# One core, attention and two MLPs: the first MLP in token chunks of 512, 256, 512, 512, 512 instead of four of 464 and one of 448, with one tanh buffer

## The chip, the cores and the metric

The kernel runs on one core of a Trainium2 chip. The metric is the device time of one execution in microseconds; the median of three runs is 832.08 (832.0 to 832.1).

## What is computed

The reference, cut to what matters, with inputs q, k, v (4, 8, 576, 64), s (4, 8, 576) and all in float32:

```python
def _attn_ref(q, k, v, s):
    scores = np.matmul(q, k.transpose(0, 1, 3, 2)) / np.sqrt(D)
    cum = np.cumsum(np.maximum(s, 0.0), axis=-1)
    bias = -(cum[:, :, :, None] - cum[:, :, None, :])
    scores = np.where(causal, -1e9, scores + np.minimum(bias, 0.0))
    attn = softmax(scores)
    return np.matmul(attn, v)

def _moe_ref(x, w_in, w_out):           # 2304 tokens, 512 -> 2048 -> 512
    h = x @ w_in
    g = h - np.tanh(h)
    return g @ w_out

def _moe2_ref(x, w_in, w_out, g_ln):    # 2304 tokens, 512 -> 1024 -> 512
    h = x @ w_in
    solu = h * softmax(h)
    ln = (solu - mean(solu)) / np.sqrt(var(solu) + 1e-6) * g_ln
    return ln @ w_out
```

The output of the attention, 4 x 576 = 2304 tokens of 512 features, goes through the first MLP (`_moe_ref`, MLP1 below) and then the second.

## The kernel before

All data of the MLPs stays in SBUF with features on the partitions: `xT` holds the 2304 tokens as four blocks of 128 features. Every product in full precision is made of three float32r matmuls, high x high, low x high and high x low, where the high part is a copy rounded to float32r (ACT) and the low part is what is left (DVE, sometimes POOL).

**MLP1** goes over the tokens in five chunks (`NCH`): with `CH = 464` (line 76) four chunks of 464 tokens and a last one of 448. The hidden layer has `FT` = 16 blocks of 128 features; a step is one block j of one chunk c, and u = 16 c + j counts the steps. The program of each engine is written out by hand, and engines meet at semaphores only:

- TensorE: `up` (L1440 to L1452) makes one block of h, 12 matmuls into PSUM bank j % 4; `down` (L1454 to L1466) adds the block's share of the output to the four banks 4 to 7, 12 matmuls. Each matmul has its own weight load of 128x128. `chunk` (L1468) orders them: in chunk 0 `down(j - 4)` before `up(j)`, in the others `up(j)` before `down(j - 2)`. The first four `up` of chunk 0 are laid between the last matmuls of the attention (`first_up`, L1484).
- ACT, `step` (L836): tanh of the bank into `gate`, high part of the gate into `gate_hi`.
- DVE, `step` (L1130): h - tanh(h) into `gate` (L1134), low part into `gate_lo` (L1146).
- `gate`, `gate_hi` and `gate_lo` have two buffers each, taken in turn by j. Tanh of step u waits for `gate_lo` of step u - 2, since that reads the same `gate` last; `gate_hi` waits for the `down` of step u - 2:

```python
act.wait_ge(up_done, u + 1)
wait(act, gate_lo_done, u - 1)
act.activation(gate[j % 2][:, 0:wide(c)], h_ps[j % 4][:, 0:wide(c)], ACT.Tanh).then_inc(tanh_done, 1)
...
act.wait_ge(gate_done, u + 1)
wait(act, down_done, u - 1)
act.activation(gate_hi[j % 2][:, 0:wide(c)], gate[j % 2][:, 0:wide(c)], ACT.Copy).then_inc(gate_hi_done, 1)
```

Between chunks ACT and DVE split the next chunk's tokens (`split_x`, L799 and L1094: four high parts, four low parts), and copy the finished chunk's output from PSUM over the tokens in `xT` (`copy_y`, L970 and L1268). The first chunk's tokens are split by POOL (`first_x`, L667) while the attention still runs.

Other work is laid into the steps of two chunks. In chunk 0 ACT and DVE split the weights of MLP1, which SP loads through four staging tiles: in step j after the tanh the parts of `w1o` (L812, L1108), after `gate_hi` and `gate_lo` one part of `w1i` (L807, L1103). In the last chunk they split the weights of the second MLP: ACT the high part in step j between tanh and `gate_hi`, DVE the low part between the subtract and `gate_lo`. `W2_STEP` (L89) says which part is in which step: B22 in 5, B11 in 6, B21 in 7 (strided reads, two instructions of 512 per engine, L825 and L1120), then four sums T4, T2, T1, T3 in 9, 10, 11, 13 (L818, L1115) and the second layer's weights in 12, 14, 15. POOL makes the four sums (L702 to L714, eight instructions), starting when `down` of step 3 of the last chunk is done; when `down` of step 9 is done it splits the first two token tiles of the second MLP (`split_y`, L716).

The second MLP follows (L1657 to L1752): `up2` makes two token tiles by seven block products (42 matmuls of 512 columns), `turn_ln` transposes, `down2` makes the output. Its first `up2` stands ahead of the last two `down` of MLP1.

Loops: the middle chunks are a loop on the chip (`Fori`), the first and the last are straight code; on ACT and DVE the last but one as well.

In SBUF the gate tiles lie at the start of the phase's area, six of `CH` words (`GATE_W`), then `w1o`, `w1i`, and the split tokens `x_hi`, `x_lo` of 4 x `CH` words each. The second MLP's tiles lie over the same area.

Of the kernel before, what the change touches and what calls it, by code (L numbers as in the profile page):

```python
# [44 lines left out]
def wait(eng, sem, count):  # L45

    if not (isinstance(count, int) and count <= 0):
        eng.wait_ge(sem, count)


def build_transformer(nc, q, k, v, s, w_in, w_out, w2_in, w2_out, g_ln, out):
# [21 lines left out]
    FT = FF // P  # L73
    FF2 = w2_in.shape[1]
    FT2 = FF2 // P
    CH = 464
    NCH = -(-TOK // CH)
    LAST_CH = TOK - (NCH - 1) * CH
    TT = TOK // P
    assert D == 64 and TAIL == 64 and FULL == 4 and H % 2 == 0 and HALVES == KT == 4 and PAIRS % 2 == 0  # L80
    assert 0 < LAST_CH <= CH and LAST_CH % 16 == 0 and NCH > 3
    assert TT * P == TOK and TT % 4 == 2 and TT > 6 and FF2 == 2 * BANK and DM == BANK and FT2 == 8

    HK = KT // 2
# [39 lines left out]
    with ctx:  # L124
# [7 lines left out]
        g_col = sb("g_col", [P, FT2])  # L132


        GATE_W = 6 * CH
        attention_words = []
        with ExitStack() as phase:
            sb = tensors(phase, attention_words)
            qkT_hi = [sb(f"qkT_hi{n}", [P, QK_W], F32R) for n in range(2)]
            qkT_lo = [sb(f"qkT_lo{n}", [P, QK_W], F32R) for n in range(2)]  # L140
            probs = [sb(f"probs{n}", [P, PW]) for n in range(2)]
            pT_hi = sb("pT_hi", [P, 2, PT_W], F32R)

            v_parts = [sb(f"v_parts{n}", [P, NT, 4 * D], F32R) for n in range(2)]
            ident_b = sb("ident_b", [P, P], BF16)
            mask_b = sb("mask_b", [P, P], BF16)
            upper_b = sb("upper_b", [P, TAIL], BF16)
            lower_b = sb("lower_b", [P, TAIL], BF16)
            tail_mask_b = sb("tail_mask_b", [P, TAIL], BF16)
            neg_max = [sb(f"neg_max{n}", [P, TILES]) for n in range(2)]  # L150
            row_sum = [sb(f"row_sum{n}", [P, TILES]) for n in range(2)]
            den = [sb(f"den{n}", [P, TILES]) for n in range(2)]
            small_b = sb("small_b", [P, 1])
            rden = [sb(f"rden{n}", [P, TILES]) for n in range(2)]
            rden_row = sb("rden_row", [TILES, P])

            w1i_words = GATE_W + FT * 2 * DM
            sb("gap", [P, w1i_words - sum(attention_words)])
            cum_bc = [sb(f"cum_bc{n}", [P, 2, S]) for n in range(2)]
            cum_tail = sb("cum_tail", [P, S])  # L160
            v_raw = [sb(f"v_raw{n}", [P, NT, 2 * D]) for n in range(2)]
            pT_lo = sb("pT_lo", [P, 2, PT_W], F32R)
            rden_T = [sb(f"rden_T{n}", [P, S]) for n in range(2)]
            qk_flat = [sb(f"qk_flat{n}", [P, FULL * P]) for n in range(2)]
            x_low = sb("x_low", [P, S])
            x_sum = sb("x_sum", [P, S])
# [10 lines left out]

        AHEAD = 4
        behind_words = AHEAD * 2 * KT * P
        before = GATE_W + FT * 2 * DM  # L180
        pad = 0
        assert sum(attention_words) <= before + FT * 2 * KT * P - behind_words
        with ExitStack() as phase:
            sb = tensors(phase)
            gate = [sb(f"gate{n}", [P, CH]) for n in range(2)]
            gate_hi = [sb(f"gate_hi{n}", [P, CH], F32R) for n in range(2)]
            gate_lo = [sb(f"gate_lo{n}", [P, CH], F32R) for n in range(2)]
            w1o = sb("w1o", [P, FT, 2, DM], F32R)
            w1o_hi, w1o_lo = ([w1o[:, j, part, :] for j in range(FT)] for part in range(2))
            w1i = sb("w1i", [P, FT, 2, KT, P], F32R)  # L190
            w1i_hi, w1i_lo = ([w1i[:, (j - AHEAD) % FT, part, :, :] for j in range(FT)] for part in range(2))
            x_hi = sb("x_hi", [P, KT, CH], F32R)
            x_lo = sb("x_lo", [P, KT, CH], F32R)

        W1O_AT, W1I_AT = GATE_W, GATE_W + FT * 2 * DM
        mlp2_words = []
        with ExitStack() as phase:
            sb = tensors(phase, mlp2_words)  # L200
            out_sb = [sb(f"out_sb{n}", [P, DM]) for n in range(2)]
            sb("pad2", [P, W1O_AT - sum(mlp2_words)])
            w2o_a = sb("w2o_a", [P, 6, 2, DM], F32R)
            y_split_a = sb("y_split_a", [P, 2, 7, HK, P], F32R)
            y_sum = sb("y_sum", [P, 2, HK, P])
            act2 = [sb(f"act2_{n}", [P, FF2]) for n in range(2)]
            lnT_hi = [sb(f"lnT_hi{n}", [P, FT2, P], F32R) for n in range(2)]
            lnT_lo = [sb(f"lnT_lo{n}", [P, FT2, P], F32R) for n in range(2)]
            assert sum(mlp2_words) == W1I_AT
            w2x = sb("w2x", [P, FT, 2, BANK], F32R)  # L210
            y_split_b = sb("y_split_b", [P, 2, 7, HK, P], F32R)
            small = sb("small", [P, 64])
# [141 lines left out]

        def wide(c):

            return LAST_CH if isinstance(c, int) and c == NCH - 1 else CH

        def tokens(c):

            return slice(c * CH, c * CH + wide(c)) if isinstance(c, int) else bass.ts(c, CH)

        def w1o_at(j):

# [424 lines left out]
        def _(act):  # L789
# [46 lines left out]
            def step(c, j):  # L836
                u = FT * c + j
                act.wait_ge(up_done, u + 1)
                wait(act, gate_lo_done, u - 1)
                act.activation(gate[j % 2][:, 0:wide(c)], h_ps[j % 4][:, 0:wide(c)], ACT.Tanh).then_inc(tanh_done, 1)  # L840
                if isinstance(c, int) and c == 0:
                    for n in w1o_at(j):
                        w1o_hi_part(n)

                if isinstance(c, int) and c == NCH - 1:
                    for name in W2_STEP:
                        if W2_STEP[name] == j:
                            w2i_hi_part(name)
                    for f in W2O_STEP.get(j, ()):
                        w2o_hi_part(f)  # L850
                act.wait_ge(gate_done, u + 1)
                wait(act, down_done, u - 1)
                act.activation(gate_hi[j % 2][:, 0:wide(c)], gate[j % 2][:, 0:wide(c)], ACT.Copy).then_inc(gate_hi_done, 1)  # L853
                if isinstance(c, int) and c == 0 and 0 < j <= FT - AHEAD:
                    w1i_hi_part(j + AHEAD - 1)

# [113 lines left out]
            def copy_y(c):  # L970
                act.wait_ge(down_done, FT * (c + 1))
                for m in range(2):
                    act.activation(xT[:, m, tokens(c)], y_ps[m][:, 0:wide(c)], ACT.Copy).then_inc(y_act, 1)
# [8 lines left out]
                    act.wait_ge(x_done, PAIRS)  # L982
                step(0, j)
            split_x(1)
            with act.Fori(1, NCH - 2) as c:
                copy_y(c - 1)
                for j in range(FT):
                    step(c, j)
                split_x(c + 1)
            copy_y(NCH - 3)  # L990
            for j in range(FT):
                step(NCH - 2, j)
            split_x(NCH - 1)
# [81 lines left out]
        def _(dve):  # L1075
# [54 lines left out]
            def step(c, j):  # L1130
                u = FT * c + j
                dve.wait_ge(tanh_done, u + 1)
                n = wide(c)
                dve.tensor_tensor(gate[j % 2][:, 0:n], h_ps[j % 4][:, 0:n], gate[j % 2][:, 0:n],  # L1134
                                  ALU.subtract).then_inc(gate_done, 1)
                if isinstance(c, int) and c == 0:
                    for m in w1o_at(j):
# [1 line left out]
                if isinstance(c, int) and c == NCH - 1:  # L1139
# [3 lines left out]
                    for f in W2O_STEP.get(j, ()):  # L1143
                        w2o_lo_part(f)
                dve.wait_ge(gate_hi_done, u + 1)
                dve.tensor_tensor(gate_lo[j % 2][:, 0:n], gate[j % 2][:, 0:n], gate_hi[j % 2][:, 0:n].bitcast(F32),  # L1146
                                  ALU.subtract).then_inc(gate_lo_done, 1)
                if isinstance(c, int) and c == 0 and 0 < j <= FT - AHEAD:
                    w1i_lo_part(j + AHEAD - 1)
# [123 lines left out]
            for j in range(1, FT):  # L1273
                step(0, j)
            split_x(1)
            with dve.Fori(1, NCH - 2) as c:
                copy_y(c - 1)
                for j in range(FT):
                    step(c, j)
                split_x(c + 1)  # L1280
            copy_y(NCH - 3)
            for j in range(FT):
                step(NCH - 2, j)
            split_x(NCH - 1)
            copy_y(NCH - 2)
            for j in range(FT):
                step(NCH - 1, j)

# [143 lines left out]
        def _(pe):  # L1432
# [219 lines left out]

            pe.wait_ge(x_added, 2 * PAIRS)
            chunk(0, True)
            with pe.Fori(1, NCH - 1) as c:
                chunk(c, False)
            def up2(i, par, n, after):  # L1657

# [116 lines left out]
```

## Time and profile before

| | us |
|---|---|
| median of three runs | 832.08 |
| profiled execution | 825.32 |
| its span, first to last instruction | 823.5 |
| PE busy | 800.8 (97%) |
| DVE busy | 475.8 (58%) |
| ACT busy | 394.7 (48%) |
| POOL busy | 280.3 (34%) |
| attention, with the first weights (to 204.85) | 204.85 |
| MLP1, from its first matmul to the second MLP's second block (204.85 to 625.39) | 420.54 |
| rest of the second MLP (625.39 to 823.5) | 198.11 |

A row of a group names line, engine, operation, the tile written, the tiles read, the shapes and the count; "busy, mean ns" are the time of the group and of one instruction. A matmul's listed duration overlaps with the next one's, so the distance between starts is what one costs. The idle time of an engine stands with what released it.

### The profile page before, as it was taken

The page shows a single profiled execution, that of the slowest core. Times are in us where ns is not written, and L with a number is a line of the kernel's source. Part 1 is how long each engine was busy: PE and PEld are TensorE (multiplying, and loading weights), DVE is VectorE, ACT ScalarE, POOL GpSimd, SP SyncE. Part 2 cuts the span into 40 slices and gives each one's busy share as a digit, 9 for nine tenths or more (in the row PEclk, how much of TensorE's full clock was granted, in tenths as well). Part 3 has the DMA queues.
Part 4 walks back from the last instruction along what each step waited for, and adds up shares of the span by engine and source line. Part 5 has one row for each costly group of instructions (what it writes and reads, how often), then busy time and mean ns, then how long its engine had stood idle before and what let it go on. Part 6 is the DMA issues. An engine that isn't in the chain of part 4 may idle for free. (4 is left out here: it accounts for less than half of the span.)

```text
span 823.5 us, 14650 instructions
## 1 busy us (share of the span) xinstructions
PE 800.8 (97%) x4498; PEld 694.6 (84%) x4498; DVE 475.8 (58%) x1101; ACT 394.7 (48%) x935; POOL 280.3 (34%) x322
## 2 busy tenths in 40 slices
PE   6999999998999999999999999998999899999998
PEld 5888888887888888888888888897888788888886
DVE  5889888888854332233223322338678666666662
ACT  5999899888544332222222222325444443433433
POOL 3687787778100000000000000008274744444400
PEclk9999999999999999999999999999999999999999
DMA  7665555545433100000000000000200000000001
GB/s 184 149 154 159 143 137 154 144 114 145 138 113 110 65 1 0 1 1 0 0 0 0 0 0 0 0 1 1 102 1 1 27 25 27 14 25 25 13 25 51
DMA packets 77719, 46.34 MB, mean 56 GB/s; under 512 B 59824, under 2 KB 68144, under 8 KB 77680
## 3 DMA queue, kind: packets, MB, share of 16 engines
q1 hardware_dynamic: 75232, 45.19, 19.3%
q10 hardware_dynamic: 2448, 0.66, 0.4%
q8 instruction: 20, 0.33, 0.2%
q14 instruction: 19, 0.16, 0.1%
HBM read 40.97 MB, written 4.87 MB: 56 GB/s over the span
## 5 line engine op out<-in xcount | busy, mean ns | idle before, releaser
L1450 PE MATMUL psum<-x_hi,w1i 128*128 128x464 f32 (+1 forms) x640 | 185.7, 371 | 0.5 <-DVE w1i L1103 0.5
L1463 PE MATMUL psum<-gate_hi,w1o 128*128 128x464 f32 (+1 forms) x640 | 146.8, 371 | 3.3 <-DVE gate_lo L1146 3.3
L1463 PEld LDWEIGHTS psum<-gate_hi,w1o 128*128 128x128 f32 x640 | 119.9, 188 | 18.0 <-DVE gate_lo L1146 4.4
L1450 PEld LDWEIGHTS psum<-x_hi,w1i 128*128 128x128 f32 x640 | 119.7, 188 | 15.0 <-DVE w1i L1103 0.9
L1146 DVE TENSOR_TENSOR gate_lo<-gate,gate_hi 128x464 fp32r<-128x464 f32 (+1 forms) x80 | 56.4, 705 | 129.7 <-ACT gate_hi L853 129.7
L853 ACT ACTIVATE gate_hi<-gate 128x464 fp32r<-128x464 f32 (+1 forms) x80 | 47.1, 589 | 154.5 <-PE psum L1463 133.6
L706 POOL TENSOR_TENSOR w2t<-stage 128x512 f32<-128x512 f32 x2 | 4.8, 2442 | 338.0 <-PE psum L1463 338.0
L1450 PE MATMUL psum<-x_lo,w1i 128*128 128x464 f32 (+1 forms) x320 | 118.7, 371 | 0.0
L1134 DVE TENSOR_TENSOR gate<-psum,gate 128x464 f32<-128x464 f32 (+1 forms) x80 | 50.8, 636 | 94.2 <-ACT gate L840 94.1
L840 ACT ACTIVATE gate<-psum 128x464 f32<-128x464 f32 (+1 forms) x80 | 44.1, 551 | 101.7 <-PE psum L1450 97.2
L878 ACT ACTIVATE probs<-probs,neg_max 128x128 f32<-128x128 f32 (+2 forms) x144 | 83.7, 587 | 10.3 <-DVE neg_max L1179 10.0
L1162 DVE TENSOR_TENSOR pT_lo<-psum,pT_hi 128x512 fp32r<-128x512 f32 (+3 forms) x160 | 72.5, 477 | 14.2 <-ACT pT_hi L869 13.3
L1463 PE MATMUL psum<-gate_lo,w1o 128*128 128x464 f32 (+1 forms) x320 | 80.0, 371 | 0.0
L869 ACT ACTIVATE pT_hi<-psum 128x512 fp32r<-128x512 f32 (+3 forms) x160 | 64.2, 435 | 9.2 <-PE psum L1582 8.6
L1721 PE MATMUL psum<-w2o_a,lnT_hi 128*128 128x512 f32 x216 | 67.6, 394 | 0.2 <-DVE lnT_lo L1372 0.2
L1179 DVE CUSTOM_DVE_ANT_0 probs<-psum,cum_bc 128x128 f32<-128x128 f32 (+3 forms) x128 | 58.5, 481 | 13.9 <-PE psum L1510 10.5
L1450 PEld LDWEIGHTS psum<-x_lo,w1i 128*128 128x128 f32 x320 | 60.1, 188 | 6.7
L1463 PEld LDWEIGHTS psum<-gate_lo,w1o 128*128 128x128 f32 x320 | 60.1, 188 | 6.4
L1582 PE MATMUL psum<-ident,probs 128*128 128x128 f32 x400 | 60.4, 279 | 0.6 <-ACT probs L878 0.5
L1549 PE MATMUL psum<-pT_hi,v_parts 128*128 128x128 f32 (+2 forms) x192 | 56.2, 331 | 1.8 <-DVE x_sum L1202 1.3
L1688 PE MATMUL psum<-w2x,y_split_a 128*128 128x512 f32 x210 | 49.6, 392 | 0.0
L1582 PEld LDWEIGHTS psum<-ident,probs 128*128 128x128 f32 x400 | 45.3, 142 | 4.6 <-ACT qk_flat L904 1.7
(154 smaller groups left out, 1421.1 us busy)
## 6 DMA issues: line engine op xcount, KB each, us to landing
cum_bc<-cum_dram SPq DMA_DIRECT2D x16, 576.0 KB, 4.7
rden_T<-rden_dram SPq DMA_DIRECT2D x32, 144.0 KB, 3.0
out_x<-out_sb SPq DMA_DIRECT2D x18, 256.0 KB, 2.0
stage<-in_q SPq DMA_DIRECT2D x32, 128.0 KB, 2.4
v_raw<-in_v SPq DMA_DIRECT2D x32, 128.0 KB, 3.6
stage<-in_moe_w_in SPq DMA_DIRECT2D x16, 256.0 KB, 3.0
stage<-in_moe_w_out SPq DMA_DIRECT2D x16, 256.0 KB, 3.4
stage<-in_k SPq DMA_DIRECT2D x28, 128.0 KB, 2.3
```

Of the source, the lines that this page charges most:

```text
L869: hi = act.activation(to(pT_hi), ps, ACT.Copy)
L878: act.activation(probs[par][:, at:at + width], probs[par][:, at:at + width], ACT.Exp, bias=neg_max[par][:, col:col + 1], scale=-1.0, accum ...
L1134: dve.tensor_tensor(gate[j % 2][:, 0:n], h_ps[j % 4][:, 0:n], gate[j % 2][:, 0:n], ALU.subtract).then_inc(gate_done, 1)
L1146: dve.tensor_tensor(gate_lo[j % 2][:, 0:n], gate[j % 2][:, 0:n], gate_hi[j % 2][:, 0:n].bitcast(F32), ALU.subtract).then_inc(gate_lo_done, 1)
L1162: lo = dve.tensor_tensor(to(pT_lo), ps, to(pT_hi).bitcast(F32), ALU.subtract)
L1179: dve.tensor_tensor_reduce(probs[par][:, at:at + width], tail_bank(sl) if h is None else score_ps[h][t], cum_tail[:, :] if h is None else ...
L1450: mm = pe.matmul(h_ps[j % 4][:, 0:wide(c)], wp[j][:, kt, :], xp[:, kt, 0:wide(c)], start=(n == 0), stop=(n == 3 * KT - 1))
L1463: mm = pe.matmul(y_ps[m][:, 0:wide(c)], wp[j][:, m * P:(m + 1) * P], gp[j % 2][:, 0:wide(c)], start=(j == 0 and wp is w1o_hi and gp is gat ...
L1549: mm = pe.matmul(x_ps[:, c0:c1], v_parts[par][:, j, 2 * h * D:2 * h * D + P], pp[:, h, j * STEP + c0:j * STEP + c1], start=(j == 0 and n = ...
L1582: mm = pe.transpose(ps[:, n * P:(n + 1) * P], probs[par][:, at:at + P], ident[:, :])
L1688: mm = pe.matmul(h2_ps[n][at], yp[:, of, kt, :], wp[:, kt, :], start=(nth == at and kt == 0 and k == 0), stop=(last and kt == HK - 1 and k ...
L1721: mm = pe.matmul(out_ps[par], lp[par][:, f, :], wp[f][:, :], start=(f == 0 and n == 0), stop=(f == FT2 - 1 and n == 2))
```

## The change

The chunk width becomes 512, one PSUM bank, and the second chunk takes the 256 tokens that are left. `tokens` moves the start of every later chunk by 256. `gate` has one buffer, so that tanh of step u waits for `gate_lo` of step u - 1. The loops begin one chunk later: TensorE's chunk 1 is straight code and chunks 2 and 3 loop; on ACT and DVE chunks 0, 1 and 4 are straight code, and `copy_y(c)` moves from the start of the next turn of the loop to the end of its own. The gate area is five of 512 words, with 48 words of padding between `w1o` and `w1i`.

```diff
-    CH = 464
+    CH = BANK
     NCH = -(-TOK // CH)
-    LAST_CH = TOK - (NCH - 1) * CH
+    SHORT = TOK - (NCH - 1) * CH
...
-        GATE_W = 6 * CH
+        GATE_W, W1_PAD = 5 * CH, 48
...
-            gate = [sb(f"gate{n}", [P, CH]) for n in range(2)]
+            gate = sb("gate", [P, CH])
...
         def wide(c):
-            return LAST_CH if isinstance(c, int) and c == NCH - 1 else CH
+            return SHORT if isinstance(c, int) and c == 1 else CH
         def tokens(c):
-            return slice(c * CH, c * CH + wide(c)) if isinstance(c, int) else bass.ts(c, CH)
+            if not isinstance(c, int):
+                return bass.ds(c * CH - (CH - SHORT), CH)
+            at = c * CH - (CH - SHORT) * (c > 1)
+            return slice(at, at + wide(c))
...
             def step(c, j):
                 u = FT * c + j
                 act.wait_ge(up_done, u + 1)
-                wait(act, gate_lo_done, u - 1)
-                act.activation(gate[j % 2][:, 0:wide(c)], h_ps[j % 4][:, 0:wide(c)], ACT.Tanh).then_inc(tanh_done, 1)
+                wait(act, gate_lo_done, u)
+                act.activation(gate[:, 0:wide(c)], h_ps[j % 4][:, 0:wide(c)], ACT.Tanh).then_inc(tanh_done, 1)
...
             split_x(1)
-            with act.Fori(1, NCH - 2) as c:
-                copy_y(c - 1)
+            copy_y(0)
+            for j in range(FT):
+                step(1, j)
+            split_x(2)
+            copy_y(1)
+            with act.Fori(2, NCH - 1) as c:
                 for j in range(FT):
                     step(c, j)
                 split_x(c + 1)
-            copy_y(NCH - 3)
-            for j in range(FT):
-                step(NCH - 2, j)
-            split_x(NCH - 1)
-            copy_y(NCH - 2)
+                copy_y(c)
             for j in range(FT):
                 step(NCH - 1, j)
...
             chunk(0, True)
-            with pe.Fori(1, NCH - 1) as c:
+            chunk(1, False)
+            with pe.Fori(2, NCH - 1) as c:
                 chunk(c, False)
```

The same edits stand in DVE's program, and the padding once more in the second MLP's area.

## Rows read from the trace of the kernel before

**Rows 1.** Stages: start:end, us, busy us (count) by engine, PE clock, DMA, GB/s.

```profile
291.29:372.17 80.88, 80.88 (x386) 72.06 (x385) 23.97 (x38) 21.32 (x38) 0.00 (x0) 1.00 0.00 1
...
533.93:625.39 91.46, 88.13 (x427) 79.72 (x426) 61.12 (x72) 37.47 (x61) 41.39 (x33) 1.00 0.07 24
```

**Rows 2.** Waits of PE: us in total, times, longest us.

```profile
PE psum L1463 <- DVE gate_lo L1146: 3.3, 3, 1.7
...
PE psum L1450 <- DVE w1i L1103: 0.5, 1, 0.5
```

**Rows 3.** Timeline of PE, chunk 4: start, us; three steps apart.

```profile
589.10 1.76 PE L1463 MATMUL psum<-gate_hi,w1o 128*128 128x448 f32 x8
...
603.67 1.81 PE L1463 MATMUL psum<-gate_hi,w1o 128*128 128x448 f32 x8
```

**Rows 4.** Chain of waits in the second MLP: start, us, what.

```profile
722.68 6.82 PE psum L1688 x30
729.50 8.16 PE psum L1721 x36
737.66 0.87 PE psum L1704 x8
```

**Rows 5.** Timeline of PE in the attention, then the weight loads of L1524.

```profile
111.02 0.42 PE L1524 MATMUL psum<-qkT_hi 128*128 128x288 f32 x2
...
111.81 0.20 PE L1526 MATMUL psum<-tail_mask_b,ident_b 128*128 128x64 bf16 x1
...
113.07 0.25 PE L1549 MATMUL psum<-pT_hi,v_parts 128*128 128x192 f32 x1
...
113.28 0.21 PE L1549 MATMUL psum<-pT_hi,v_parts 128*128 128x64 f32 x1
...
L1524 PEld LDWEIGHTS psum<-qkT_hi,qkT_lo 128*128 128x128 f32 x32 | 5.2, 189 | 0.0
```

**Rows 6.** Groups by line and shape on ACT and DVE: busy us, mean ns, idle before.

```profile
L853 ACT ACTIVATE gate_hi<-gate 128x464 fp32r<-128x464 f32 x64 | 37.8, 591 | 130.8 <-PE psum L1463 122.9 <-DVE gate L1134 7.8
L840 ACT ACTIVATE gate<-psum 128x464 f32<-128x464 f32 x64 | 35.5, 554 | 81.7 <-PE psum L1450 79.0 <-DVE gate_lo L1146 2.7
...
L1146 DVE TENSOR_TENSOR gate_lo<-gate,gate_hi 128x464 fp32r<-128x464 f32 x64 | 41.1, 642 | 121.3 <-ACT gate_hi L853 121.3
L1134 DVE TENSOR_TENSOR gate<-psum,gate 128x464 f32<-128x464 f32 x64 | 40.9, 639 | 79.1 <-ACT gate L840 79.0
...
L1134 DVE TENSOR_TENSOR gate<-psum,gate 128x448 f32<-128x448 f32 x16 | 10.0, 622 | 15.1 <-ACT gate L840 15.1
```

**Rows 7.** Timeline of ACT, chunk 4, steps 5 and 6.

```profile
556.02 0.54 ACT L840 ACTIVATE gate<-psum 128x448 f32<-128x448 f32 x1 [1.78 <-PE psum L1450]
...
561.31 2.38 ACT L825 ACTIVATE w2x<-stage 128x512 fp32r<-128x512 f32 x2
```

**Rows 8.** Timeline of DVE, chunk 4, steps 5 to 7.

```profile
558.79 5.57 DVE L1120 TENSOR_TENSOR w2x<-stage,w2x 128x512 fp32r<-128x512 f32 x2 [1.57 <-ACT w2x L825]
564.28 2.02 DVE L1146 TENSOR_TENSOR gate_lo<-gate,gate_hi 128x448 fp32r<-128x448 f32 x1
...
566.77 4.54 DVE L1120 TENSOR_TENSOR w2x<-stage,w2x 128x512 fp32r<-128x512 f32 x2
571.24 1.90 DVE L1146 TENSOR_TENSOR gate_lo<-gate,gate_hi 128x448 fp32r<-128x448 f32 x1
...
578.60 0.62 DVE L1146 TENSOR_TENSOR gate_lo<-gate,gate_hi 128x448 fp32r<-128x448 f32 x1
```

**Rows 9.** Timeline of POOL, first and last of the sums.

```profile
558.57 4.84 POOL L706 TENSOR_TENSOR w2t<-stage 128x512 f32<-128x512 f32 x2 [337.96 <-PE psum L1463]
...
572.62 5.17 POOL L714 TENSOR_TENSOR w2t<-stage 128x512 f32<-128x512 f32 x2
```

**Rows 10.** Stages early in the attention, columns as in rows 1.

```profile
15.00:19.50 4.50, 2.34 (x27) 1.62 (x26) 2.61 (x8) 3.64 (x10) 2.28 (x3) 1.00 0.67 153
19.50:23.00 3.50, 3.50 (x20) 2.73 (x19) 2.87 (x15) 2.88 (x12) 2.24 (x4) 0.51 0.89 250
```

More of the change, by code:

```diff
@@ L75, in build_transformer @@
     FT2 = FF2 // P
-    CH = 464
+    CH = BANK
     NCH = -(-TOK // CH)
-    LAST_CH = TOK - (NCH - 1) * CH
+    SHORT = TOK - (NCH - 1) * CH
     TT = TOK // P
     assert D == 64 and TAIL == 64 and FULL == 4 and H % 2 == 0 and HALVES == KT == 4 and PAIRS % 2 == 0
-    assert 0 < LAST_CH <= CH and LAST_CH % 16 == 0 and NCH > 3
+    assert 0 < SHORT <= CH and SHORT % P == 0 and NCH == 5
     assert TT * P == TOK and TT % 4 == 2 and TT > 6 and FF2 == 2 * BANK and DM == BANK and FT2 == 8
@@ L155, in build_transformer @@
             rden_row = sb("rden_row", [TILES, P])
-            w1i_words = GATE_W + FT * 2 * DM
+            w1i_words = GATE_W + FT * 2 * DM + W1_PAD
             sb("gap", [P, w1i_words - sum(attention_words)])
@@ L179, in build_transformer @@
         behind_words = AHEAD * 2 * KT * P
-        before = GATE_W + FT * 2 * DM
+        before = GATE_W + FT * 2 * DM + W1_PAD
         pad = 0
@@ L189, in build_transformer @@
             w1o_hi, w1o_lo = ([w1o[:, j, part, :] for j in range(FT)] for part in range(2))
+            sb("pad1", [P, W1_PAD])
             w1i = sb("w1i", [P, FT, 2, KT, P], F32R)
@@ L193, in build_transformer @@
             x_lo = sb("x_lo", [P, KT, CH], F32R)
-        W1O_AT, W1I_AT = GATE_W, GATE_W + FT * 2 * DM
+        W1O_AT, W1I_AT = GATE_W, before
         mlp2_words = []
@@ L208, in build_transformer @@
             lnT_lo = [sb(f"lnT_lo{n}", [P, FT2, P], F32R) for n in range(2)]
+            sb("pad4", [P, W1_PAD])
             assert sum(mlp2_words) == W1I_AT
@@ L852, in step @@
                 wait(act, down_done, u - 1)
-                act.activation(gate_hi[j % 2][:, 0:wide(c)], gate[j % 2][:, 0:wide(c)], ACT.Copy).then_inc(gate_hi_done, 1)
+                act.activation(gate_hi[j % 2][:, 0:wide(c)], gate[:, 0:wide(c)], ACT.Copy).then_inc(gate_hi_done, 1)
                 if isinstance(c, int) and c == 0 and 0 < j <= FT - AHEAD:
@@ L1133, in step @@
                 n = wide(c)
-                dve.tensor_tensor(gate[j % 2][:, 0:n], h_ps[j % 4][:, 0:n], gate[j % 2][:, 0:n],
+                dve.tensor_tensor(gate[:, 0:n], h_ps[j % 4][:, 0:n], gate[:, 0:n],
                                   ALU.subtract).then_inc(gate_done, 1)
@@ L1145, in step @@
                 dve.wait_ge(gate_hi_done, u + 1)
-                dve.tensor_tensor(gate_lo[j % 2][:, 0:n], gate[j % 2][:, 0:n], gate_hi[j % 2][:, 0:n].bitcast(F32),
+                dve.tensor_tensor(gate_lo[j % 2][:, 0:n], gate[:, 0:n], gate_hi[j % 2][:, 0:n].bitcast(F32),
                                   ALU.subtract).then_inc(gate_lo_done, 1)
@@ L1275, in _ @@
             split_x(1)
-            with dve.Fori(1, NCH - 2) as c:
-                copy_y(c - 1)
+            copy_y(0)
+            for j in range(FT):
+                step(1, j)
+            split_x(2)
+            copy_y(1)
+            with dve.Fori(2, NCH - 1) as c:
                 for j in range(FT):
@@ L1280, in _ @@
                 split_x(c + 1)
[L1281 to L1285, printed above, removed]
+                copy_y(c)
             for j in range(FT):
```

## Prediction, made blind

> **What bounds the kernel now.** I read the stages first. The first MLP (MLP1) is one unbroken stretch of TensorE work: chunks 1, 2 and 3 take 80.88 us each (three rows alike, one shown) with PE busy for all of it, at a granted clock of 1.00, while DVE and ACT are busy for under a third [rows 1]. Each chunk holds 16 x 24 = 384 matmuls, so a 464-wide one costs 80.88/384 = 0.2106 us from start to start. Only chunk 4 shows PE short of its window (88.13 of 91.46) [rows 1]. The waits of PE name the cause: three waits for gate_lo in the down product, 3.3 us together; and one of 0.5 us for a w1i part in chunk 0 [rows 2]. So time moves by what one matmul costs at the new widths, and by what happens to the three stalls.
>
> **Matmul cost by width.** Four widths can be read as pitches.
> - 464: 0.2106 us (above).
> - 448: in the quiet part of chunk 4, three steps of 24 take 603.67 - 589.10 = 14.57 us, 0.2024 each [rows 3].
> - 512: in the second MLP 30 take 6.82 us (0.2273) and 36 take 8.16 us (0.2267) [rows 4]. I use 0.2270.
> - 256 appears with fp32 weights of 128x128 nowhere. Nearest above it: six of 288 take 111.81 - 111.02 = 0.79 us, 0.1317 each. Nearest below: two of 192 start in 113.28 - 113.07 = 0.21 us, 0.105 each [rows 5].
>
> The line through 288 and 512 rises (0.2270 - 0.1317)/224 = 0.000425 us per column; at 256 it gives 0.118. Bounds: not below the 192-wide 0.105, not above the 288-wide 0.1317. I take 0.119, near the line, because 288 is the closer of the two neighbours. The same line gives 0.2066 at 464 and 0.1998 at 448, so the present widths lie 0.0040 and 0.0026 above it: that excess is the whole of what can be won.
>
> **The change, part by part.**
>
> Chunks 0, 2, 3, from 464 to 512: each 384 x 0.2270 = 87.17, in place of 80.88, +6.29; three make +18.9. (Chunk 0 is mixed with the last attention work, but has the same 384 matmuls.)
>
> Chunk 1, from 464 to 256: 384 x 0.119 = 45.7 in place of 80.88, -35.2. By the bounds 40.3 to 50.6, so -5.4 to +4.9 around it.
>
> Chunk 4, from 448 to 512: 87.17 in place of 384 x 0.2024 = 77.7, +9.5.
>
> Together **-6.8 us**. A 512 pitch as high as 0.231 (the 464's extra 0.0040 added) would add 384 x 4 x 0.004 = 6.1.
>
> One tanh buffer. tanh of unit j now waits for gate_lo of j-1, not j-2; behind it on ACT stand gate_hi and, in chunks 0 and 4, the weight parts; DVE's subtract waits for it. Where nothing else is in the chain, tanh, subtract, gate_hi, gate_lo take 0.554 + 0.639 + 0.591 + 0.642 = 2.43 us at 464 [rows 6]; the step rate of PE is 24 x 0.2106 = 5.05. From 464 to 448 the subtract loses (639 - 622)/16 = 1.06 ns per column [rows 6]; with that for all four the chain is at most 2.63 at 512 against a step of 5.45, and about 1.55 at 256 against 2.86. Two further steps of slack stand behind it, since down(j) is issued after up(j+2). Cost zero in chunks 1 to 3; the cover is PE's step, and without it each step would cost the difference to the chain. In chunk 0 ACT has a w1o and a w1i part per step, but those still fit, and PE's longer first products cover part of the 0.5 us wait [rows 2]: I take -0.3, bounds -0.5 and +0.5.
>
> Boundary from chunk 1 to 2. Before it PE runs three downs of the short chunk, 36 x 0.119 = 4.3 us; in that time ACT must finish gate_hi(15) and four 512-wide x_hi copies, the first startable after one down (1.4) and gate_hi (0.4 at this width), then four copies of the length of gate_hi's row [rows 6], about 0.6: 1.8 + 2.5 = 4.3. Nothing to 0.3; I take +0.2. All others keep 36 x 0.227 = 8.2 us of cover. The order copy_y, steps, split_x on ACT and DVE is the same as before, only cut differently into loop and straight code; POOL's first x parts and the y copies grow by 0.1 to 0.2 each beside PE. SP's queue has no moved issue. POOL's weight sums still start at the fourth down of chunk 4, its token splits at the tenth: both keep their lead, as steps get longer. I take 0 for these.
>
> **Chunk 4, the one place where the buffer matters.** Steps 5, 6, 7 split the strided halves B22, B11, B21 of the second MLP's weights. Now: tanh(5) starts at 556.02, ACT makes the high parts, DVE's two low parts begin at 558.79 (2.77 later), take until 564.28 (5.49), and gate_lo(5) lasts 2.02 [rows 7, 8]. ACT meanwhile has tanh(6) and the high parts of B11 ready by 563.7, long before DVE is free, so DVE's next low parts start at 566.77, half a microsecond after gate_lo(5) [rows 7, 8]. With one buffer tanh(6) must wait for that gate_lo, so the 2.8 us from tanh to the first low part stand in the chain, in steps 6 and 7. Set tanh(5) at 0:
> - gate_lo(5) ends at 10.3, plus 0.2 for width: 10.5. PE reaches down(5) at 4 x 12 x 0.227 - 0.2 = 10.7: the first stall goes.
> - tanh(6) 10.5, low parts 13.3, two of them 4.5 to 5.5 [rows 8], gate_lo 1.9 to 2.0: ends 19.7 to 20.8. PE gets there at 10.7 + 5.45 = 16.2: a stall of 3.5 to 4.6 (1.9 by starts now; 1.7 listed [rows 2]).
> - tanh(7) about 20.3, low parts 23.1. POOL's sums, which run beside DVE from 558.57 to 577.79 [rows 9], would end at 22.1. After them gate_lo took 0.62, beside them 1.90 and 2.02 [rows 8]; the low parts beside them 4.5 to 5.5. Alone they lie between a third of 5, 1.6, and 5.0. I take 2.6, nearer the ratio of the gate_lo rows: gate_lo(7) ends 26.4, PE wants it at 25.7: 0.7, bounds 0 and 3.1.
> - tanh(8) starts 0.6 late, but no weight part is in step 8 and PE has two products to go: nothing.
>
> Stalls of chunk 4 now: 91.46 - 77.7 - 42 x 0.2270 (the first product block of the second MLP, inside the window) = 4.2. After: 4.0 + 0.7 + 0.4 of small change = 5.1, bounds 3.9 and 8.1. **+1.0 us**, from -0.3 to +3.9.
>
> Sum: -6.8 - 0.3 + 0.2 + 1.0 = -5.9, and +0.1 for wider y copies in the next stage's chain: **-5.8 us**. The profiled execution took 825.32 (span 823.5 and 1.8 around it), so 819.5; the median of the runs, 832.08, is 6.8 above the profiled one, and I carry that over: **826.3**.
>
> **Rivals.**
>
> A. The excess of 464 and 448 belongs to the stage, not to the width: every MLP1 matmul pays the same fixed part above its columns. The count (1920) and the columns (2304) are unchanged, so the matmuls win nothing, and stalls and boundary leave +1.0: 833.1, no change or just slower. For it: those two widths stand only in MLP1's rows here. Against it: the excess differs inside the stage, 0.0040 at 464 with quiet engines and 0.0026 at 448 beside the weight work of chunk 4, so it goes with the width rather than with traffic. The Trainium skill, "TensorE: Matmul & The Clock Gate", section "Back-to-back issue gap", gives the gap as the columns over 2.4 GHz plus a constant 2.5 ns; by it this rival holds exactly, yet its constant is below what every row here shows. 11%.
>
> B. The short chunk is bound by its weight loads. Every matmul has its own, and the rows list 189 ns for one [rows 5]. If 256 columns no longer hid it, chunk 1 would take 384 x 0.189 = 72.6, 26.9 more: 853.2, slower. The change turns slower where the 256 pitch passes (45.7 + 5.8)/384 = 0.134. Against it: 288-wide ones start every 0.132 with the same listed load, and eight transposes, each with a new load, take 0.87, 0.109 each [rows 4, 5]; that floor is below 0.119. 5%.
>
> C. Chunk 4 loses more: stalls at 8.1, and PE's clock falls in the longer gap. The trace shows one fall: granted 0.51 from 19.5 to 23, after a stretch in which PE was busy 2.34 of 4.5 us [rows 10]. Such a stretch costs 3.5 x 0.5 = 1.7. In chunk 4 now it stays at 1.00 [rows 1]. With +2.9 and 1.7: 826.3 + 4.6 = 830.9. The Trainium skill's same page, section "Why this matters for your kernels", warns that idle gaps between bursts bring the low clock back; no run shows it at this length of gap. 12%.
>
> **Numbers.** The forecast has 72%. Its own range: 512 and 256 pitches and the stall bounds give 823 to 829.5. To hold eight in ten I extend to C: 823.0 to 831.0, leaving out A, B and the far ends. About 0.2% (1.7 us) is what a measurement can tell here. Faster: the forecast and part of C, with rests of A: 0.80. Same: most of A and some of C: 0.12. Slower: B and the ends of A: 0.08.
>
> **What would show it.** Chunks 0, 2, 3, 4 at 0.227 per matmul, chunk 1 some 46 us long without gaps; in chunk 4 the wait at down(5) gone, the one at down(6) near 4 us, tanh(6) and tanh(7) right behind gate_lo(5) and (6). The forecast is wrong if 512-wide ones of MLP1 need 0.230 or more, if chunk 1 takes over 51 us, or if chunk 4's gate_lo waits pass 8 us.

## The result, and the profile after

| | before | after |
|---|---|---|
| median of 12 runs each, measured side by side, us | 827.54 (825.24 to 832.85) | 822.85 (820.29 to 825.51) |
| lowest run, us | 825.24 | 820.29 |
| profiled execution, us (granted clock, mean) | 825.32 (0.998) | 824.0 (0.994) |

The ratio of the times is 0.9935, with a 95% interval of 0.9911 to 0.9959: faster by about 0.65%, some 5 us. The 12 runs of before take in the three known ahead of the prediction (832.0 to 832.1); these lie at the upper end.

The two profiled executions differ by 1.3 us only, since their clocks differ. The page of after:

```profile
span 822.2 us, 14626 instructions
...
PE 800.8 (97%) x4498; PEld 670.5 (82%) x4498; DVE 471.5 (57%) x1101; ACT 396.2 (48%) x935; POOL 280.4 (34%) x322
```

Its stages follow, in the view by stretches with the columns of [rows 1]: the end of the attention, then chunks 0 to 4 (the last with the first product block of the second MLP), then a stretch of the second MLP.

```profile
203.00:206.38 3.38, 3.38 (x17) 3.22 (x16) 2.52 (x4) 0.74 (x2) 3.11 (x3) 0.50 0.16 62
206.38:299.46 93.08, 92.97 (x422) 76.66 (x420) 49.52 (x78) 39.79 (x74) 2.87 (x2) 1.00 0.30 94
299.46:345.10 45.64, 45.64 (x386) 45.59 (x384) 16.55 (x37) 15.99 (x38) 0.00 (x0) 1.00 0.00 1
345.10:432.99 87.89, 87.89 (x387) 72.18 (x386) 26.12 (x40) 22.45 (x38) 0.00 (x0) 1.00 0.00 1
432.99:520.77 87.78, 87.78 (x385) 72.08 (x384) 25.89 (x38) 22.88 (x38) 0.00 (x0) 1.00 0.00 0
520.77:620.72 99.95, 98.10 (x427) 79.78 (x426) 58.24 (x72) 39.18 (x61) 41.59 (x34) 1.00 0.06 22
...
643.30:646.80 3.50, 2.87 (x11) 2.68 (x12) 2.02 (x7) 1.65 (x3) 1.81 (x3) 0.51 0.20 75
```

Chunk 0's row before, which [rows 1] does not show:

```profile
204.85:291.29 86.44, 85.91 (x422) 76.60 (x421) 48.24 (x79) 37.68 (x74) 4.02 (x3) 1.00 0.33 102
```

What to see. The short chunk takes 45.64 us in place of 80.88 [rows 1], a wide one 87.8 to 87.9. Chunk 0's window was 86.44 us and grew by 6.6; chunk 4's was 91.46 [rows 1] and grew by 8.5. The five together went from 420.5 to 414.3: -6.2. Against that stand two stretches at half clock, at 203.0 and 643.3, that the profile of before has not (both have the one near 19 [rows 10]). The first costs about 1.5 us (the attention ends at 206.38 in place of 204.85). The second costs about 1.3, since PE stands still for the first part of it. Without these two the profiled execution of after would take about 821.2 (an estimate), 4.1 below that of before; the medians differ by 4.7. The spread goes with the clock as well: the run of after at 820.29 has a mean clock of 1.000, the one at 825.51 one of 0.993.

The rest is in the second MLP, from the end of chunk 4's window to the end of the span: it grew from 198.1 to 201.5. The chain of waits shows where. Before, and then after:

```profile
648.61 1.09 PE psum L1704 x8
649.71 2.75 PE psum L1721 x12
...
656.06 6.85 PE psum L1688 x30
```

```profile
643.93 1.97 PE psum L1711 x8
645.90 3.23 PE psum L1728 x12
...
652.81 7.00 PE psum L1695 x30
...
659.81 8.25 PE psum L1728 x36
...
675.34 6.87 PE psum L1695 x30
...
682.20 8.24 PE psum L1728 x36
```

The first two rows of each are the fall of the clock: 5.2 us against 3.8. From the x30 row to the end of the span after takes 822.2 - 652.8 = 169.4, and before 823.5 - 656.1 = 167.4: the other 2.0. There, the rows of before are 6.82 to 6.86 for x30 and 8.16 for x36 [rows 4]. Work that the change doesn't touch has become slower, up to 7.00/30 = 0.2333 against 0.2273 per matmul.

PE's wait for gate_lo in MLP1 after, where before has 3.3, 3, 1.7 [rows 2]. The wait of 0.5 us for a w1i part is no longer in the list:

```profile
PE psum L1469 <- DVE gate_lo L1152: 1.9, 2, 1.2
```

Steps 5 to 7 of chunk 4 after, in the timelines of DVE, ACT, PE and POOL (to be read beside [rows 7, 8, 9]):

```profile
548.47 3.92 DVE L1126 TENSOR_TENSOR w2x<-stage,w2x 128x512 fp32r<-128x512 f32 x2 [1.52 <-ACT w2x L831]
552.32 2.43 DVE L1152 TENSOR_TENSOR gate_lo<-gate,gate_hi 128x512 fp32r<-128x512 f32 x1
...
557.67 3.57 DVE L1126 TENSOR_TENSOR w2x<-stage,w2x 128x512 fp32r<-128x512 f32 x2 [1.51 <-ACT w2x L831]
561.16 2.04 DVE L1152 TENSOR_TENSOR gate_lo<-gate,gate_hi 128x512 fp32r<-128x512 f32 x1
...
566.14 2.87 DVE L1126 TENSOR_TENSOR w2x<-stage,w2x 128x512 fp32r<-128x512 f32 x2 [1.52 <-ACT w2x L831]
568.94 0.67 DVE L1152 TENSOR_TENSOR gate_lo<-gate,gate_hi 128x512 fp32r<-128x512 f32 x1
```

```profile
545.62 0.60 ACT L846 ACTIVATE gate<-psum 128x512 f32<-128x512 f32 x1 [2.04 <-PE psum L1456]
...
554.84 0.60 ACT L846 ACTIVATE gate<-psum 128x512 f32<-128x512 f32 x1 [5.76 <-DVE gate_lo L1152]
```

```profile
563.26 2.11 PE L1469 MATMUL psum<-gate_hi,w1o 128*128 128x512 f32 x8 [1.19 <-DVE gate_lo L1152]
...
569.67 2.11 PE L1469 MATMUL psum<-gate_hi,w1o 128*128 128x512 f32 x8 [0.66 <-DVE gate_lo L1152]
```

```profile
548.52 5.67 POOL L712 TENSOR_TENSOR w2t<-stage 128x512 f32<-128x512 f32 x2 [325.67 <-PE psum L1469]
...
562.61 4.45 POOL L720 TENSOR_TENSOR w2t<-stage 128x512 f32<-128x512 f32 x2
```

Tanh(6) now starts 0.1 us after gate_lo(5) ends, and ACT waited 5.76 us for it: the new wait is there. Yet PE waits only at down(6) and down(7). From start to start these two matmuls take 1.6 and 1.0 us, 2.2 more than two normal pitches, and the matmul behind each takes another 0.1: chunk 4 has 2.4 us of stalls where it had 4.2.

### The profile page after: what moved, and what is told of

Its sections match the earlier page's. It is cut to its first block and busy times, and to the rows that moved or that the text cites. A ratio compares the mean times of both kernels' runs of the same rounds, so it can differ in the third digit from the quotient of the medians.

```text
span 822.2 us, 14626 instructions
## 1 busy us (share of the span) xinstructions
PE 800.8 (97%) x4498; PEld 670.5 (82%) x4498; DVE 471.5 (57%) x1101; ACT 396.2 (48%) x935; POOL 280.4 (34%) x322
## 5 line engine op out<-in xcount | busy, mean ns | idle before, releaser
L1456 PE MATMUL psum<-x_hi,w1i 128*128 128x512 f32 (+1 forms) x640 | 182.0, 369 | 0.1
L1469 PE MATMUL psum<-gate_hi,w1o 128*128 128x512 f32 (+1 forms) x640 | 146.2, 370 | 1.9 <-DVE gate_lo L1152 1.9
L1456 PEld LDWEIGHTS psum<-x_hi,w1i 128*128 128x128 f32 x640 | 115.6, 188 | 20.8 <-DVE w1i L1109 0.5
L1469 PEld LDWEIGHTS psum<-gate_hi,w1o 128*128 128x128 f32 x640 | 112.3, 188 | 23.7 <-DVE gate_lo L1152 2.7
L1152 DVE TENSOR_TENSOR gate_lo<-gate,gate_hi 128x512 fp32r<-128x512 f32 (+1 forms) x80 | 55.4, 692 | 123.0 <-ACT gate_hi L859 122.9
L1456 PE MATMUL psum<-x_lo,w1i 128*128 128x512 f32 (+1 forms) x320 | 117.7, 368 | 0.0
L859 ACT ACTIVATE gate_hi<-gate 128x512 fp32r<-128x512 f32 (+1 forms) x80 | 47.2, 590 | 132.1 <-PE psum L1469 123.2
L1140 DVE TENSOR_TENSOR gate<-psum,gate 128x512 f32<-128x512 f32 (+1 forms) x80 | 51.0, 638 | 94.7 <-ACT gate L846 93.1
L846 ACT ACTIVATE gate<-psum 128x512 f32<-128x512 f32 (+1 forms) x80 | 44.4, 555 | 117.0 <-PE psum L1456 86.8
L1469 PE MATMUL psum<-gate_lo,w1o 128*128 128x512 f32 (+1 forms) x320 | 79.2, 369 | 0.0
```

Source lines behind the costliest of these rows:

```text
L1140: dve.tensor_tensor(gate[:, 0:n], h_ps[j % 4][:, 0:n], gate[:, 0:n], ALU.subtract).then_inc(gate_done, 1)
L1152: dve.tensor_tensor(gate_lo[j % 2][:, 0:n], gate[:, 0:n], gate_hi[j % 2][:, 0:n].bitcast(F32), ALU.subtract).then_inc(gate_lo_done, 1)
L1456: mm = pe.matmul(h_ps[j % 4][:, 0:wide(c)], wp[j][:, kt, :], xp[:, kt, 0:wide(c)], start=(n == 0), stop=(n == 3 * KT - 1))
L1469: mm = pe.matmul(y_ps[m][:, 0:wide(c)], wp[j][:, m * P:(m + 1) * P], gp[j % 2][:, 0:wide(c)], start=(j == 0 and wp is w1o_hi and gp is gat ...
```

## The experiments

Besides the cut into loops, three things changed together: the widths, the number of tanh buffers, and the addresses of all MLP tiles, since `GATE_W` is another number and `W1_PAD` moves what lies behind it by 48 words. Theories: **width** (464 and 448 carry an excess per matmul that 512 and 256 don't), **place** (pitches follow the addresses), **buffer** (the tanh wait costs little). All kernels below compute the full result. The runs of before beside them had medians of 826.97 (29 runs; for e1, e3, e4 and e6) and 826.50 (11; for e2, e5, e9 and e10). No run has two tanh buffers at 512 columns, so what the buffer costs at that width was not measured by itself.

**One buffer alone (e4_onebuf).** Before, widths and places kept:

```diff
-            gate = [sb(f"gate{n}", [P, CH]) for n in range(2)]
+            gate = sb("gate", [P, CH])
+            sb("spare", [P, CH])
...
-                wait(act, gate_lo_done, u - 1)
+                wait(act, gate_lo_done, u)
```

> The kernel before with one tanh buffer, the second's place left empty, so that no address moves; widths 464 and 448. Theory 'one buffer exposes ACT's tanh and high parts in steps 6 and 7 of chunk 4': the wait at the down product of step 5 stays near 0.8 us, the one at step 6 grows from 1.9 to about 4, the one at step 7 is 1 to 2: in sum 2 to 3 us more than before, 0.3% slower. Rival 'DVE's low parts beside POOL set the pace, not the buffer': the three waits stay within 0.5 us of the sum before, no change. Chunks 1 to 3 stay at 80.9 us each in both.

Measured: 830.11 us, ratio 1.0039 (1.0025 to 1.0053): slower by 3.1. The chunks in the loop keep 80.88. In chunk 4, first DVE's, ACT's and PE's timelines, then the stretches:

```profile
570.26 3.49 DVE L1121 TENSOR_TENSOR w2x<-stage,w2x 128x512 fp32r<-128x512 f32 x2 [1.70 <-ACT w2x L826]
573.67 2.35 DVE L1147 TENSOR_TENSOR gate_lo<-gate,gate_hi 128x448 fp32r<-128x448 f32 x1
```

```profile
567.36 0.54 ACT L841 ACTIVATE gate<-psum 128x448 f32<-128x448 f32 x1 [7.16 <-DVE gate_lo L1147]
```

```profile
576.08 3.35 PE L1464 MATMUL psum<-gate_hi,w1o 128*128 128x448 f32 x8 [3.64 <-DVE gate_lo L1147]
```

```profile
572.00:574.80 2.80, 0.45 (x3) 0.08 (x1) 2.80 (x2) 0.00 (x0) 2.80 (x2) 0.99 0.00 0
574.80:581.60 6.80, 5.52 (x15) 4.92 (x16) 4.49 (x5) 3.19 (x5) 3.18 (x2) 0.50 0.01 2
```

PE stands still for 3.6 us, from 572.4 to 576.1. The clock falls at 574.8, inside this wait, and stays at half for 6.8 us. PE works for 5.5 us of that; its matmuls there come every 0.373 us in place of 0.203, and this costs about 2.7. The waits by themselves are hardly longer than in before: beyond normal pitches 0.8 at down(5) and 3.8 at down(6), where before has 0.8, 1.9 and 1.1 at down(5) to down(7); the one at down(7) doesn't show behind the half clock. So the expected sum came out (3.1 for 2 to 3), but most of it is the clock and not, as the expectation had it, the waits. At 448 the one buffer does what rival C said of 512: a long wait and a fall of the clock. "Buffer costs little" doesn't hold for the old widths.

**The old widths in the new layout (e1_464_in_512).** After, with 464-wide chunks and a last one of 448 in the 512-wide tiles (ACT's and DVE's loops are written out here):

```diff
-    SHORT = TOK - (NCH - 1) * CH
+    USED = 464
+    SHORT = TOK - (NCH - 1) * USED
...
-            return SHORT if isinstance(c, int) and c == 1 else CH
+            return SHORT if isinstance(c, int) and c == NCH - 1 else USED
```

> The changed kernel's tiles (512 columns wide, one tanh buffer, same addresses), but the token chunks of the kernel before: four of 464 and one of 448. Theory 'width': a 464-column matmul carries its extra 0.004 us wherever its operands lie, so chunks 1 to 3 stay at 80.9 us each (0.2106 per matmul), and the time is that of the kernel before plus what one tanh buffer costs. Rival 'address': the extra belongs to where the operands lie in SBUF (tiles 464 words apart, in place of 512), so in 512-wide tiles the 464-column matmul falls to about 0.207 to 0.208, chunks 1 to 3 to 79.5 to 79.9 us each, and the time lies within 2 us of the changed kernel's. Both: the products of the second MLP keep the slower pace of the changed kernel (30 in 6.87 to 7.01 us), as its tiles lie where they lie there.

Measured: 831.37 us, ratio 1.0048 (1.0031 to 1.0064). A chunk's stretch, and PE's wait:

```profile
371.75:452.18 80.43, 80.43 (x386) 72.10 (x385) 23.95 (x38) 21.34 (x38) 0.00 (x0) 1.00 0.00 1
```

```profile
PE psum L1469 <- DVE gate_lo L1152: 6.5, 2, 5.8
```

464 costs 80.43/384 = 0.2094 here, against 0.2106 [rows 1]: the layout moves it by 0.0012, where the rival wanted 0.0026 to 0.0036. One wait of 5.8 comes from a low pair that took 7.52 us beside POOL's sums; inside it the clock falls, to half for 6.8 us. With the old widths everything else of the change makes the kernel slower.

**All MLP tiles at equal places (e3_all40).** In after w1o starts 8 words behind a multiple of 64, and w1i, w2x and the split tokens 56 behind one; before has all of them at 40. Here the change keeps its widths and its one buffer, and gets the places of before:

```diff
-        GATE_W, W1_PAD = 5 * CH, 48
+        LEAD, W1_PAD = 96, 0
+        GATE_W = 5 * CH + LEAD
...
+            sb("pad0", [P, LEAD])
```

> The changed kernel with 96 words in front of the gate tiles and none between w1o and w1i, so that every tile of both MLPs starts at the same place within 64 words as in the kernel before (40 past a multiple). Theory 'address': the changed kernel's 512-column matmuls take 0.2286 in the first MLP and 0.233 for some products of the second because w1o and what follows it start 48 words apart in that count; here all fall to 0.2270 or below: chunks 2 and 3 to 87.2 us from 87.8, the second MLP's 30 products to 6.82 us from 6.87 to 7.01, together 4 us off the changed kernel, a ratio to the kernel before of 0.988 to 0.990. Rival 'the width or the stage sets it': paces as in the changed kernel, ratio 0.9935.

Measured: 818.59 us, ratio 0.9900 (0.988 to 0.992), 4.3 below after. Chunks 1 and 3, then the chain in the second MLP:

```profile
298.38:344.46 46.08, 46.08 (x385) 46.03 (x384) 16.55 (x37) 15.99 (x38) 0.00 (x0) 1.00 0.00 1
...
431.63:518.67 87.04, 87.04 (x385) 72.10 (x384) 25.89 (x38) 22.85 (x38) 0.00 (x0) 1.00 0.00 0
```

```profile
649.88 6.84 PE psum L1695 x30
...
656.73 8.16 PE psum L1728 x36
```

87.04/384 = 0.2267, and the second MLP is back at [rows 4]. The parts: 4 x 384 x (0.2286 - 0.2267) = 2.9 in MLP1, less 0.4 for the short chunk, and 2.0 in the second MLP: 4.5, against 4.3 by the medians.

**The old widths at equal places (e9_464_all40).** The last two edits together.

> Token chunks of 464 and 448 in 512-wide tiles that all start 40 words past a multiple of 64, as in the version with all tiles at 40, where a 512-column matmul takes 0.2267. Theory 'width': 464 keeps an extra of its own even with the best addresses, 0.209 or more per matmul, chunks 1 to 3 at 80.3 us or more each. Rival 'address': on the line through 288 and 512 columns it falls to 0.2066, chunks 1 to 3 to 79.3 us. Both: the second MLP's products at 0.227; the long wait at the down product of step 6 of chunk 4 (5.8 us in the run with 464 columns before) is there again, 4 to 6 us, as it depends on the one tanh buffer and the shorter step.

Measured: 830.58 us, ratio 1.0046 (1.0030 to 1.0063). A chunk of 464:

```profile
373.49:454.13 80.64, 80.64 (x386) 71.95 (x384) 23.96 (x38) 21.36 (x38) 0.00 (x0) 1.00 0.00 1
```

PE's wait:

```profile
PE psum L1469 <- DVE gate_lo L1152: 6.6, 2, 5.9
```

464 costs 0.2100 and 448 0.2027 where 512 and 256 in the same layout cost 0.2267 and 0.1200. Beside the columns at 2.4 GHz (193.3, 186.7, 213.3, 106.7 ns) that leaves 16.7 and 16.0 ns against 13.4 and 13.3. Width held; place is not the reason for 464's excess. The long wait is there again, as expected, and with it 6.8 us at half clock.

**Before with the 48 words put in (e5_before_pad48).**

```diff
-        GATE_W = 6 * CH
+        GATE_W, W1_PAD = 6 * CH, 48
...
+            sb("pad1", [P, W1_PAD])
```

> The kernel before with 48 words put between w1o and w1i (and in the second MLP's area), nothing else. Theory 'address': the second MLP's products of w2x with the first token tile and with lnT rise from 0.2277 and 0.2268 to about 0.233, those of w2o with lnT stay at 0.2273, so the second MLP gets 1.5 to 2 us longer, with no width changed. Rival 'the slower second MLP of the changed kernel comes from the chunks or from the buffer': no product changes its pace by over 0.0005.

Measured: 830.61 us, ratio 1.0044 (1.0027 to 1.0061). The chain in the second MLP:

```profile
659.94 7.00 PE psum L1690 x30
...
666.94 8.25 PE psum L1723 x36
```

The same 7.00 and 8.25 as in after, from the 48 words alone. Chunks of 464 stay at 80.73, so a 464-wide product doesn't mind the pad and a 512-wide one does. The products account for about 2 of the 4.1 us. The profiled execution also has three falls of the clock, at 9.8, 204.3 and 651.5 us, that the one of before has not; the last alone costs about 1.4. The rest of the 4.1 is put down to such falls, which the trace of one execution can't show for the others.

**All tiles at another equal place (e2_all8).** As e3_all40, with `LEAD` of 64, which puts all at 8.

> The changed kernel with 64 words in front and none between w1o and w1i: all tiles of both MLPs start 8 words past a multiple of 64. Theory 'a matmul is slow when its two operands start differently within 64 words': the second MLP's products of w2x with the first token tile and with lnT fall from 0.233 to 0.2285 or less, those that already agreed (w2o, gates) stay at 0.2282 to 0.2302. Rival 'each tile has its own good place and 8 is a bad one': w2x products stay at 0.233 and x products of the first MLP rise from 0.2275 to 0.229 or more.

Measured: 820.09 us, one run. A wide chunk:

```profile
434.08:521.12 87.04, 87.04 (x386) 72.07 (x384) 25.89 (x38) 22.86 (x38) 0.00 (x0) 1.00 0.00 0
```

Equal to e3_all40 to the last digit: between these two places it makes no difference, while 48 words between the groups do. One point went against me: in after the gate tiles and w1o lie at 8 together, as here, and still their products took 0.2302 there and 0.2268 here. So the two operands of a matmul do not explain it by themselves; what does is open.

**High parts ahead of tanh (e6_hi_first).** In steps 5 to 7 of after ACT makes the high parts before it waits for gate_lo, so that the new wait no longer delays DVE:

```diff
+                if isinstance(c, int) and c == NCH - 1:
+                    for name in W2_STEP:
+                        if W2_STEP[name] == j and name[0] == "B":
+                            w2i_hi_part(name)
                 wait(act, gate_lo_done, u)
```

> The changed kernel with ACT making the high parts of B22, B11 and B21 ahead of the tanh's wait for gate_lo in steps 5, 6 and 7 of chunk 4, not behind the tanh. Theory 'tanh behind gate_lo delays the high parts, and they the low parts': DVE's low parts start 1.4 us after the tanh starts in place of 2.8, the two waits of chunk 4 (1.6 and 1.0 us from start to start) shrink by 1.4 us or more each to nearly nothing: 2 us faster than the changed kernel, ratio to the kernel before near 0.991. Rival 'the low parts only collide longer with POOL's sums when they start earlier': their time grows by what the start wins, waits unchanged.

Measured: 826.49 us (822.06 to 830.78), ratio 0.9999 (0.9975 to 1.0024). DVE's three low pairs:

```profile
548.84 5.21 DVE L1130 TENSOR_TENSOR w2x<-stage,w2x 128x512 fp32r<-128x512 f32 x2
...
557.29 3.60 DVE L1130 TENSOR_TENSOR w2x<-stage,w2x 128x512 fp32r<-128x512 f32 x2
...
564.11 4.26 DVE L1130 TENSOR_TENSOR w2x<-stage,w2x 128x512 fp32r<-128x512 f32 x2
```

The pairs now start 1.2 us after the tanh of their step in place of 2.8, but take 5.21, 3.60 and 4.26 instead of 3.92, 3.57 and 2.87; and in step 5 the tanh itself comes 2 us later, behind the high parts. What is won in the chain is mostly lost beside POOL, as the rival said: PE's waits for gate_lo are 1.5 against 1.9, and the 2 us did not come. The median is above after's, which the profiled execution (822.06) does not show. The runs above 828 have mean clocks of 0.990 to 0.992 and those below 823 have 0.995, but a run at 0.991 took 824.79, so the clock by itself doesn't sort them. None of the long ones was profiled: what makes them long is open.

**POOL's sums after the low pairs (e10_sums_late).** e3_all40 and one wait:

```diff
+            pool.wait_ge(w2i_lo_done, 3)
```

> The version with all tiles at 40, with POOL's sums held until DVE's three strided low pairs of chunk 4 are done. Theory 'the low pairs and gate_lo are slow because POOL's sums run beside them': the pairs fall from 3.9, 3.6 and 2.9 us to under 2.8 each, gate_lo of steps 5 and 6 from 2.4 and 2.0 to 0.7, the waits of PE at steps 6 and 7 (1.5 and 1.0 us from start to start) go; the sums alone take under 15 us in place of 18.5, T4 is ready at or shortly after step 9 asks for it, and the time falls by 1.5 to 2 us, ratio near 0.988. Rival 'strided reads are slow by themselves': pairs stay above 2.8 us, waits stay, and T4 comes late: 3 us or more slower than the version with all tiles at 40.

Measured: 817.78 us (816.04 to 820.13), ratio 0.9896 (0.9877 to 0.9915). DVE's timeline, and the first and last of POOL's sums:

```profile
546.92 2.20 DVE L1127 TENSOR_TENSOR w2x<-stage,w2x 128x512 fp32r<-128x512 f32 x2 [1.45 <-ACT w2x L832]
549.03 0.68 DVE L1153 TENSOR_TENSOR gate_lo<-gate,gate_hi 128x512 fp32r<-128x512 f32 x1
...
552.58 2.18 DVE L1127 TENSOR_TENSOR w2x<-stage,w2x 128x512 fp32r<-128x512 f32 x2 [1.45 <-ACT w2x L832]
```

```profile
560.59 4.28 POOL L713 TENSOR_TENSOR w2t<-stage 128x512 f32<-128x512 f32 x2 [337.43 <-DVE w2x L1127]
...
571.62 5.00 POOL L721 TENSOR_TENSOR w2t<-stage 128x512 f32<-128x512 f32 x2
```

Alone a low pair takes 2.2 us and gate_lo 0.68; PE's waits at down(6) and down(7) are gone, and one of 0.86 us from start to start comes up later, where the sums end late. The sums took 16.0 us in place of 18.5, not under 15. MLP1's last chunk gains 1.6 us in the profiles, but the medians, 818.59 and 817.78, differ by 0.8, and the ratios 0.9900 and 0.9896 lie within each other's intervals. Both beat the kernel before and the change; between them this doesn't decide.

## Where the prediction was wrong, and where it was right

The measured 822.85 lies below the stated range of 823.0 to 831.0, so the forecast of the time failed. The forecast of the change, -5.8 us or a ratio of 0.9930, lies inside the measured interval. Step by step:

| step | predicted | measured, and where |
|---|---|---|
| matmuls by width | -6.8 | -4.3 (stages; 512 at 0.2286) |
| w1i wait in chunk 0 | -0.3 | -0.4 (start to start) |
| boundary 1 to 2 | +0.2 | +0.1 (330 ns for 227) |
| stalls of chunk 4 | +1.0 | -1.8 (4.2 to 2.4) |
| second MLP | +0.1 | +2.0 (chain, without the fall) |
| sum | -5.8 | -4.4 (medians: -4.7) |

That the sum comes so near is partly luck: three terms are off by +2.5, -2.8 and +1.9 and largely cancel.

- **The step that failed is the level**: "the median of the runs, 832.08, is 6.8 above the profiled one, and I carry that over". The three runs came from the upper end of a spread of 825.2 to 832.9: beside them nine more put before at 827.54, 2.2 above the profile. So the level was 4.5 too high; the change came out 1.1 smaller than forecast, which took some of that back, and 826.3 is 3.45 above the measured median, the range's low end, 823.0, 0.15 above it. The clock of those three runs is not on record. But where it is, the same program took 825.0 to 826.5 us at a mean clock of 0.998 and 828.3 to 831.2 at 0.992, so the 6.8 is put down to falls of the clock, which belong to an execution and not to the kernel. Carrying over what the one row of a fall shows, 0 to 4 of them at 1.7, would have given 819.5 to 826.3.
- **512 in MLP1, mis-sized**: I took the 0.2270 of the second MLP; after shows 0.2286, +2.5 us over four chunks. Not the width is the reason but the 48 words, as e3_all40 shows (0.2267). The prediction put the pad at nothing, without a reason.
- **256, right**: 45.64 us, 0.1189 against 0.119 taken. The line through 288 and 512 held (0.118).
- **The excess goes with the width, right**: rival A said it belongs to the stage; e9_464_all40 and e3_all40 show 16.7 ns at 464 and 13.3 to 13.4 at 256 and 512 in one layout. The Trainium skill, "TensorE: Matmul & The Clock Gate", section "Back-to-back issue gap", by which that rival held exactly, has a constant of 2.5 ns, and gives it for one matmul by itself, which the prediction left out; no width here is that low and it is not constant. Rival B is out by the pitch: 0.1189 in the short chunk, against its 0.189. But weight loads are under way for 45.59 of the chunk's 45.64 us, where a chunk of 464 had 72.06 of 80.88 [rows 1]; no run has a narrower one, so whether the line goes on below 256 is open.
- **Chunk 4, right in place and wrong in size**: tanh(6) and tanh(7) are right behind gate_lo, the low pairs 2.83 us after tanh, the stall at down(5) is gone, as worked out. But the term "low parts 4.5 to 5.5" measured 3.92 and 3.57, and the chain from tanh(5) to the end of gate_lo(6) 563.20 - 545.62 = 17.6 where 19.7 to 20.8 was taken; PE's stall at down(6), beyond a normal pitch, is 1.4 instead of 3.5 to 4.6. (The prediction's own 5.1 less 4.2 is +0.9, not +1.0.) How long a pair takes depends on how it falls among POOL's sums: 2.2 alone (e10_sums_late), up to 7.52 beside them. The Trainium skill, "SBUF — State Buffer", section "SBUF: two separate sides", says that DVE with two SBUF inputs and GpSimd take one port pair as an exclusive lock, the other waiting until the instruction is over. The runs agree with it: 0.68 against 2.04 to 2.43 for the same gate_lo.
- **Rival C's mechanism exists**, at the old widths: e4_onebuf, e1_464_in_512 and e9_464_all40 have waits of 3.6, 5.8 and 5.9, and in each the clock falls to half for 6.8 us. In chunk 4 at 512 no wait was that long. So one buffer costs 3 us with 448 columns, most of it by the clock; at 512 the stalls are smaller than before even with one buffer. There PE comes later by half a microsecond per step and the pairs fall better among POOL's sums. How much of this is the widths and how much the luck of the phase was not separated.
- **Unforeseen**: 2.0 us in the second MLP, by the same 48 words (e5_before_pad48).

## What to carry to other kernels

Read the pitch of a matmul off a quiet stretch for every width that the kernel has, and tile so that the costliest excess is not the common case. When an edit changes the size of one tile, all tiles behind it move: look at the pitch of matmuls that the edit doesn't touch, since here 48 words between two groups took back 4.3 of 8.4 us (the gain of e3_all40). And a level is not carried over from a few runs whose clock isn't that of the profiled one: forecast the difference, and put the falls of the clock into the range.

## What was not expected of the hardware

- A 512-wide float32r matmul of MLP1 took 0.2267 us with all tile groups at the same offset from a multiple of 64 words (e3_all40, e2_all8), and 0.2274 to 0.2302 by its operands with 48 words between the groups (after); in the second MLP up to 0.2333. One of 464 moved by 0.0012 at most, one of 256 became faster (0.1189 against 0.1200).
- Per matmul 13.3 to 13.4 ns stand above the columns at 256 and 512, and 16.0 to 16.7 at 448 and 464, in one layout (e3_all40 and e9_464_all40).
- A pair of subtractions on DVE took between 2.18 and 7.52 us by what POOL did beside it.
- In a stall of PE of 3.6 us the granted clock fell to 0.50 for 6.8 us (e4_onebuf); with the stalls of up to 1.6 us from start to start in chunk 4 of the kernel after it stayed at 1.00. The length of a wait doesn't settle it: PE's wait for ACT early in the second MLP was 2.7 us in the profile of before, at a clock of 1.00, and 2.6 in that of after, with the fall at 643.3. In e4_onebuf, whose second MLP is that of before, it was 2.7 with a fall at 653.3. Before, then after:

```profile
PE psum L1704 <- ACT act L1025: 2.7, 1, 2.7
```

```profile
PE psum L1711 <- ACT act L1031: 2.6, 1, 2.6
```
